# A float32r mask in place of a bfloat16 one, put ahead of the score matmuls instead of between them

## What is computed

```python
scores = scale * q @ k.T
block_i, block_j = pos[:, None] // 64, pos[None, :] // 64
scores = where(block_i >= block_j, scores, -1e9)
attn = exp(scores - max(scores)); attn = attn / (sum(attn) + 1e-09)
x = attn @ v
for w_in, w_out, act in layers:      # clip(h+3, 0, 6)*h/6, then h*tanh(log1p(exp(h)))
    x = act(x @ w_in) @ w_out
```

## Time and profile before

| | before |
|---|---|
| median of three executions | 996.41 us (994.26 to 997.54) |
| profiled execution | 994.92 us, span of the trace 993.1 us |
| PE busy | 963.6 us, 97% of the span, 6132 matmuls |
| PEld busy | 858.2 us, 6132 loads |
| DVE, ACT, POOL busy | 759.8, 648.4, 464.0 us |
| stage of attention | from 8.5 to about 207 us |
| mask matmuls (L747) | 128, first at 8.8 us, last at 205.8 us |

### The profile page before, as it was taken

The page is one execution under the profiler, slowest core; times in us unless marked ns, Lnnn a source line. Parts: engine busy times, 40 slices in busy tenths (PEclk is TensorE's granted clock), DMA queues, the critical chain, the costliest instruction groups (busy, mean ns, idle before and its releaser), DMA issues.

```text
span 993.1 us, 17891 instructions
## 1 busy us (share of the span) xinstructions
PE 963.6 (97%) x6132; PEld 858.2 (86%) x6132; DVE 759.8 (77%) x1283; ACT 648.4 (65%) x1429; POOL 464.0 (47%) x441
## 2 busy tenths in 40 slices
PE   6999999999999999999999999999999999999998
PEld 5887888899888888998889999899899898998996
DVE  5998888878686866879797786876877877776654
ACT  6888888856555554544445556777777777776663
POOL 7888899967676576968686680000000000000000
PEclk9999999999999999999999999999999999999999
DMA  6778867564689978587977545546645645465255
GB/s 160 211 189 228 222 167 200 151 172 147 221 286 318 321 257 288 182 290 274 316 245 256 199 153 188 222 158 229 219 170 205 230 178 194 170 232 195 93 186 197
DMA packets 81914, 211.49 MB, mean 213 GB/s; under 512 B 12320, under 2 KB 19104, under 8 KB 81824
## 3 DMA queue, kind: packets, MB, share of 16 engines
q1 hardware_dynamic: 81744, 210.06, 65.0%
q10 hardware_dynamic: 80, 0.29, 0.1%
HBM read 170.39 MB, written 39.92 MB: 212 GB/s over the span
## 4 chain that ended last, share of the span: by engine, by line
PE 87%; DVE 7%; issue 3%; ACT 2%; DMA 1%; POOL 1%; SPq 0%; ACTq 0%; DVEq 0%; POOLq 0%
PE psum L956 36%; PE psum L839 11%; PE psum L840 11%; PE psum L841 11%; PE psum L789 5%; PE psum L768 5%; PE psum L744 3%; PE psum L749 3%; DVE ebuf L1519 1%; DVE glo L1525 1%; DMA ext_d<-ext_made 1%; DVE wlo L1417 1%; PE psum L747 1%; DVE ext_made L1425 1%; DMA qkin<-in_qk 1%
## 5 line engine op out<-in xcount | busy, mean ns | idle before, releaser
L956 PE MATMUL psum<-ghi,osplit 128*128 128x512 f32 (+1 forms) x640 | 215.3, 370 | 0.3 <-POOL osplit L1770 0.3
L839 PE MATMUL psum<-xhi,whi 128*128 128x256 f32 (+1 forms) x640 | 187.6, 293 | 2.0 <-ACT snap L1166 2.0
L841 PE MATMUL psum<-xhi,wlo 128*128 128x256 f32 (+1 forms) x640 | 187.5, 293 | 0.0
L840 PE MATMUL psum<-xlo,whi 128*128 128x256 f32 (+1 forms) x640 | 187.4, 293 | 0.0
L956 PE MATMUL psum<-osplit,ghi 128*128 128x512 f32 x576 | 181.2, 396 | 1.4 <-DVE glo L1525 1.4
L1525 DVE SCALAR_TENSOR_TENSOR glo<-ebuf,ghi 128x512 fp32r<-128x512 f32 x144 | 129.9, 902 | 22.5 <-ACT ghi L1214 14.2
L839 PEld LDWEIGHTS psum<-xhi,whi 128*128 128x128 f32 x640 | 121.4, 190 | 15.0 <-ACT snap L1166 3.2
L1770 POOL TENSOR_TENSOR osplit<-oraw,osplit 128x512 fp32r<-128x512 f32 x80 | 117.5, 1471 | 35.7 <-ACT osplit L1133 31.7
L956 PEld LDWEIGHTS psum<-ghi,osplit 128*128 128x128 f32 x640 | 118.1, 189 | 15.8 <-issue 0.4
L840 PEld LDWEIGHTS psum<-xlo,whi 128*128 128x128 f32 x640 | 121.2, 189 | 10.1
L1214 ACT ACTIVATE ghi<-ebuf 128x512 fp32r<-128x512 f32 x144 | 90.1, 626 | 59.4 <-DVE ebuf L1519 37.4
(11 more groups left out here) (113 smaller groups left out, 2252.2 us busy)
## 6 DMA issues: line engine op xcount, KB each, us to landing
ext<-ext_d SPq DMA_DIRECT2D x56, 768.0 KB, 4.4
osplit<-o_d SPq DMA_DIRECT2D x80, 512.0 KB, 5.2
oraw<-in_w_out SPq DMA_DIRECT2D x80, 256.0 KB, 5.8
qkin<-in_qk SPq DMA_DIRECT2D x63, 288.0 KB, 4.3
wraw<-in_w_in SPq DMA_DIRECT2D x32, 512.0 KB, 5.3
ext_d<-ext_made SPq DMA_DIRECT2D x32, 384.0 KB, 5.8
attn_t<-ostage SPq DMA_DIRECT2D x64, 144.0 KB, 3.1
o_d<-staged SPq DMA_DIRECT2D x32, 256.0 KB, 5.4
```

The lines of the kernel that those rows point to most:

```text
L839: pe.matmul(dst, hi, xh, start=(start and cc == 0), stop=False, skip_group_check=True)
L840: pe.matmul(dst, hi, xl, start=False, stop=False, skip_group_check=True)
L841: last = pe.matmul(dst, lo, xh, start=False, stop=(stop and cc == 1), skip_group_check=True)
L956: last = pe.matmul(bank(Y_BANK + c, n), stat, mov, start=(first and m == 0), stop=(final and m == 2), skip_group_check=True)
```

## The change

The mask operands become float32r. `mask_val` gets 128 columns, of which the first 64 are zero. The mask is now the first matmul of a tile and covers its last 128 columns; it carries the start flag, and `khi` follows without it. Tile 4, which has no mask, is as before. float32r operands are made by a copy, so POOL writes the raw values into `oraw[0]`, which is not in use at that time, and copies them. The mask tiles move to the part of the memory that only attention uses, and three small constants share one tensor.

```diff
-        three = sb("three", [P, 1], F32)
-        one = sb("one", [P, 1], F32)
+        small = sb("small", [P, 2 + 2 * NT], F32)
+        three, one = small[:, 0:1], small[:, 1:2]
+        negmax = [small[:, 2 + s * NT:2 + (s + 1) * NT] for s in range(2)]
         ident = sb("ident", [P, P], F32)
-        mask_rows = sb("mask_rows", [P, P], BF16)
-        mask_val = sb("mask_val", [P, DH], BF16)
-        negmax = [sb(f"negmax{s}", [P, NT], F32) for s in range(2)]
...
+            mask_rows = ab("mask_rows", [P, P], F32R)
+            mask_val = ab("mask_val", [P, P], F32R)
...
-                    pe.matmul(bank(pb, w), q_tile, khi[s][:, k0:k0 + w], start=True, stop=False)
                     if i < 4:
-
-                        pe.matmul(bank(pb, DH, PW[i] - DH), mask_rows[:, :], mask_val[:, :],
-                                  start=False, stop=False, skip_group_check=True)
-                    last = pe.matmul(bank(pb, w), q_tile, klo[s][:, k0:k0 + w], start=False, stop=True)
+                        pe.matmul(bank(pb, P, PW[i] - P), mask_rows[:, :], mask_val[:, :],
+                                  start=True, stop=False, skip_group_check=True)
+                    pe.matmul(bank(pb, w), q_tile, khi[s][:, k0:k0 + w], start=(i == 4), stop=False,
+                              skip_group_check=True)
+                    last = pe.matmul(bank(pb, w), q_tile, klo[s][:, k0:k0 + w], start=False, stop=True,
+                                     skip_group_check=True)
...
-            pe.wait_ge(consts_ready, 2)
+            pe.wait_ge(consts_ready, 3)
...
+            raw_rows, raw_val = oraw[0][:, 0:P], oraw[0][:, P:2 * P]
+            nc.gpsimd.memset(oraw[0][:, 0:P + DH], 0.0).then_inc(memset_done, 1)
+            nc.gpsimd.memset(oraw[0][:, P + DH:2 * P], MASKED).then_inc(memset_done, 1)
             nc.gpsimd.memset(ident[:, :], 0.0).then_inc(memset_done, 1)
-            nc.gpsimd.memset(mask_rows[:, :], 0.0).then_inc(memset_done, 1)
-            nc.gpsimd.memset(mask_val[:, :], MASKED).then_inc(memset_done, 1)
...
             pool.wait_ge(memset_done, 5)
+            nc.gpsimd.memset(raw_rows[0:1, 0:DH], 1.0).then_inc(memset_done, 1)
             nc.gpsimd.affine_select(out=ident[:, :], ...).then_inc(consts_ready, 1)
-            nc.gpsimd.memset(mask_rows[0:1, 0:DH], 1.0).then_inc(consts_ready, 1)
+            nc.gpsimd.tensor_copy(mask_val[:, :], raw_val).then_inc(consts_ready, 1)
+            pool.wait_ge(memset_done, 6)
+            nc.gpsimd.tensor_copy(mask_rows[:, :], raw_rows).then_inc(consts_ready, 1)
```

More of the change, by code:

```diff
@@ L9 @@
 F32R = mybir.dt.float32r
-BF16 = mybir.dt.bfloat16
 AX = mybir.AxisListType
@@ L1790, in next_x @@
                             split_x_lo(blk, cc, i)
+            raw_rows, raw_val = oraw[0][:, 0:P], oraw[0][:, P:2 * P]
+            nc.gpsimd.memset(oraw[0][:, 0:P + DH], 0.0).then_inc(memset_done, 1)
+            nc.gpsimd.memset(oraw[0][:, P + DH:2 * P], MASKED).then_inc(memset_done, 1)
             nc.gpsimd.memset(ident[:, :], 0.0).then_inc(memset_done, 1)
-            nc.gpsimd.memset(mask_rows[:, :], 0.0).then_inc(memset_done, 1)
-            nc.gpsimd.memset(mask_val[:, :], MASKED).then_inc(memset_done, 1)
-            nc.gpsimd.memset(three[:, :], 3.0).then_inc(memset_done, 1)
-            nc.gpsimd.memset(one[:, :], 1.0).then_inc(memset_done, 1)
+            nc.gpsimd.memset(three, 3.0).then_inc(memset_done, 1)
+            nc.gpsimd.memset(one, 1.0).then_inc(memset_done, 1)
             pool.wait_ge(memset_done, 5)
+            nc.gpsimd.memset(raw_rows[0:1, 0:DH], 1.0).then_inc(memset_done, 1)
             nc.gpsimd.affine_select(out=ident[:, :], in_=ident[:, :], compare_op=ALU.not_equal, fill=1.0,
                                     base=0, pattern=[[-1, P]], channel_multiplier=1).then_inc(consts_ready, 1)
-            nc.gpsimd.memset(mask_rows[0:1, 0:DH], 1.0).then_inc(consts_ready, 1)
+            nc.gpsimd.tensor_copy(mask_val[:, :], raw_val).then_inc(consts_ready, 1)
+            pool.wait_ge(memset_done, 6)
+            nc.gpsimd.tensor_copy(mask_rows[:, :], raw_rows).then_inc(consts_ready, 1)
             for n in range(FIRST, NHEAD):
```

## The result

| | before | after |
|---|---|---|
| median (executions) | 995.68 us (20) | 993.31 us (20) |
| ratio, 95% interval | | 0.9978 (0.9970 to 0.9987) |
| profiled execution, span | 994.92, 993.1 us | 995.47, 993.7 us |
| matmuls | 6132 | 6132 |

The changed kernel is 2.2 us faster (1.3 to 3.0 us, by the ratio; the medians differ by 2.4). The gain lies within 0.3%, and inside the range of 992.8 to 999.5. But it is more than the 0.6 us that was forecast, and the two profiled executions don't show it. So a single pair of spans can't say where the gain is, and means over many records have to.

A forecast was written before the change was run, and what follows sets the result against it. PE was taken to set the pace in about 17 of 32 attention heads. The profiled 994.92 us less 0.6 us gives 994.3; with the median 1.49 us above, 995.8 us was forecast, range 992.8 to 999.5.

The forecast's parts named there:

- What bounds the kernel: Whole run: PE, busy 97% of the span; in attention, PE sets the pace except in about 15 of 32 heads.
- The 17 heads: Attention: the roughly 17 of 32 heads in which PE, not DVE or POOL, was taken to set the pace.
- The mask before, 0.13 us: Attention tiles: the bfloat16 mask's load does not run under khi, so a mask costs 0.13 us of PE.
- The mask after, 0.11 us: Attention tiles: a float32r mask ahead of khi, its load hidden, costs 0.11 us like the short attend matmuls.
- The net of 0.03 us per head: Four masks per head: 0.06 us saved in three tiles, 0.03 us lost in the tile of 128 columns.
- The lost fast load: Slower rival: masks' float32 load, or khi's behind it, unhidden; 0.09 us more per mask, 6.3 to 11.8 us; chance 0.12.
- The estimate of 80 ns lost: 128 masks: giving up the skill's fast bfloat16 weight load loses 80 ns each, 10 us if nothing hid it.
- The faster rival: Attention masks: a mask costs only its columns, 0.06 us, saving 0.28 us per head, 4.8 us; chance 0.09.
- The addresses: Attention's buffers: shifted addresses change no shapes or transfer sizes; no row prices them, 1 us kept either side.
- Its last sentence: Stage from 207 us on: the prediction would be wrong if its length changed, since nothing there is touched.

The follow-up runs named there:

- two masks: The changed kernel with its float32r mask matmul issued twice in each tile: ratio 1.0028, 999.08 us; a head without a stall takes 6.18 us.
- The order run: The kernel before with only the bfloat16 mask of 64 columns put first in its tile, khi and klo behind it: ratio 0.9967, 992.85 us.
- the run with the layers' buffers put back: The changed kernel with 448 unused bytes ahead of the layers' buffers (whi4 to snap3), returning them to the addresses of the kernel before: ratio 1.0004.
- the three shifts tried: The kernel before with constants joined and masks moved (ratio 0.9979), only masks moved (4.0 us slower), or only constants joined (1 us gain).

## Why the prediction was right, and where it wasn't

**What bounds the kernel.** Right in kind. Pairs of heads that POOL paces took 12.51 to 12.56 us with the mask before, changed or left out (5.75 plus 6.81 us in the changed kernel), so that what TensorE saves there goes into the stall. This is also why no mask at all brings only 3 to 4 us over the changed kernel. The 17 heads that TensorE was said to pace were too many, since two masks show 11 to 13.

**The mask before, 0.13 us.** Its size was read rightly, its cause only half. It was put down to the bfloat16 load, which starts late. That load is short; what costs is the float32r load behind it, which starts at the mask's start and is exposed. The run without masks gives 0.12 us for it in the tiles of 256 and 384 columns. The prediction stopped at the sum for a mask in the middle of a tile and never asked what the same break would cost elsewhere. The order run shows it: 0.20 us per head less, with the load type kept.

**The mask after, 0.11 us.** Right, by the trace after and by the two masks at 0.11 us each. That its own load runs under what stands before the tile does not hold in the tile of 512 columns, where `khi`'s load was not hidden before either. The exposed load only changed its name.

**The net of 0.03 us per head.** Mis-sized by rounding differences of 0.01 us. From the loads' starts in the two traces, the tiles of 256, 384 and 512 columns saved 0.01 to 0.02 us each and the one of 128 columns lost 0.03 to 0.04. The head measures 5.74 to 5.75 us instead of the 5.72 forecast. The masks and the start are all that the run with the layers' buffers put back has left of the change, beside attention's own addresses: 1.0004 (0.9994 to 1.0014). So their 0.6 us isn't shown, and it may well be nothing.

**The lost fast load (the slower rival, 0.12).** It didn't come. The mask's load record doubled, from 98 to 194 ns, and a head didn't get longer. The shorter record fits the fast weight load that the Trainium skill describes ("TensorE: Matmul & The Clock Gate", section on weight-path performance modes). In the old place a short load gained nothing, since it was started late. The estimate of 80 ns lost took the load to be four times as fast; the records are a factor of two apart. At the head of a tile the bfloat16 type is worth having: 5.55 us with it there, 5.74 with float32r. Whether the faster load is the reason isn't shown. The sum of this rival has a slip of 0.3 us: 994.92 plus 6.3 and 11.8 is 1001.2 and 1006.7.

**The faster rival (0.09), that the change of type is what costs.** Not in the form given, since float32r masks did not fall to 0.06 us. It was near a true thing all the same: the break between the types costs, and in three of the four tiles it can be put where it costs little.

**The addresses.** This is the step that failed. The prediction said that it knew of no row that prices them and allowed 1 us to either side. They made 2.1 us here and from 4.0 slower to 2.1 faster in the three shifts tried. Its last sentence said that it would be wrong if the stage from 207 us on changed its length, "since nothing in it is touched". By that sign it was wrong: 4,700 matmuls there came closer by half a nanosecond on average, and over all traces the stage is 1.5 us shorter, though in the pair before and after stalls hide it. The number fell into the range, and the sign was right, by luck: the 2.2 us come from a part of the edit that the sum priced at nothing, and the 1 us kept for it in the range was half of what it gave. A result within 0.3% had been given 0.77, and one outcome can't say more of that than that it came.

## What to carry to other kernels

Between float32r matmuls, a bfloat16 matmul costs the load of the next weights, 0.12 to 0.13 us, which long matmuls on both sides could have hidden. Try it behind short ones, where a load is exposed or binds in any case: that made it cheap in three of four tiles here, and not in the fourth, behind transposes of 128 columns. Changing its type in place gained nothing that could be measured. An edit that moves a buffer moves everything allocated behind it, and in a kernel with thousands of matmuls that alone can be a few tenths of a per cent either way. Before such a small gain is put down to the edit, time the kernel with the addresses alone changed, and with them put back.

## What the runs showed of the hardware that was not expected

- The distance between 256-column float32r matmuls depends on where their buffers lie in a partition. For the three kinds of pairs in the table it is 116.4 to 117.7 ns at one set of addresses, 118.2 to 119.5 at another 448 bytes away, and 119.0 to 119.3 ns at a third. Several of the 512-column pairs went the other way by 2 to 3 ns, for example 227.6 to 231.0 ns from `osplit,glo` to `xhi,ext`.
- The float32r mask costs 0.11 us with 128 or 64 columns, in front of its tile or within it. The bfloat16 mask costs 0.12 to 0.13 us within the tiles of 256 and 384 columns. Put first, it costs 0.02 us in the tile of 512 columns, 0.04 in that of 384 and 0.11 in that of 256.
